# The first four expert tiles of a recurrence-and-router kernel loaded in rows and transposed by TensorE

## What is computed

```python
sig = 1.0 / (1.0 + np.exp(-f_logit))
f = lower_bound + (1.0 - lower_bound) * sig
for t in range(S):
    h = f[:, t] * h + (1.0 - f[:, t]) * x[:, t]
    y[:, t] = h
# router on y, as 20224 rows of 256
logits = normalized(y) @ normalized(expert_emb).T / tau
e = argmax(logits)
gate = softmax(logits)[e]
out = gate * (relu(y @ w1[e]) @ w2[e])    # w1: 256x1024, w2: 1024x256
```

## Time and profile before

| | us |
|---|---|
| median of three executions | 477.56 |
| lowest, highest of the three | 477.22, 479.57 |
| the profiled execution's own time | 479.34 |
| its span, first to last instruction | 477.5 |
| TensorE busy (93% of the span) | 442.5 |
| VectorE busy (75%) | 358.7 |
| GpSimd busy (70%) | 332.0 |
| ScalarE busy (68%) | 323.9 |

### The profile page before, as it was taken

How to read it: one execution, slowest core, us unless ns; L and a number is a source line. 1 busy time by engine, 2 the same in 40 slices (tenths; PEclk the granted TensorE clock), 3 DMA queues, 4 the chain that set the end, 5 groups by cost and what they waited for, 6 DMA issues and landing times. The chain is left out here.

```text
span 477.5 us, 12371 instructions
## 1 busy us (share of the span) xinstructions
PE 442.5 (93%) x4082; PEld 378.3 (79%) x4082; DVE 358.7 (75%) x1075; ACT 323.9 (68%) x567; POOL 332.0 (70%) x388
## 2 busy tenths in 40 slices
PE   7975868869999999999999999999999999999994
PEld 4554555657898888898887869999999999988993
DVE  6997899967999999999999999654455455444542
ACT  4886878975889989999988964444454454434441
POOL 8154657735777777777777777777777777777654
PEclk9998899997999999999999999999999999999998
DMA  7999999999999999999999654565554546455511
GB/s 235 310 330 316 256 317 327 216 220 312 306 258 295 277 304 295 288 326 259 289 262 225 141 125 115 143 145 130 133 126 124 132 108 134 113 141 138 110 63 67
DMA packets 122081, 100.44 MB, mean 210 GB/s; under 512 B 100052, under 2 KB 101087, under 8 KB 122016
## 3 DMA queue, kind: packets, MB, share of 16 engines
q1 hardware_dynamic: 104064, 59.33, 49.3%
q0 software_dynamic: 16224, 40.26, 31.9%
q10 hardware_dynamic: 1728, 0.01, 0.2%
HBM read 58.37 MB, written 32.93 MB: 191 GB/s over the span
## 5 line engine op out<-in xcount | busy, mean ns | idle before, releaser
L1465 POOL DMA_INDIRECT out_dram<-osb,xm x162 | 160.6, 992 | 63.3 <-issue 36.8
L1106 POOL DMA_INDIRECT XsScratch<-Yt,sli x158 | 152.3, 964 | 65.4 <-issue 23.8
L1440 PE MATMUL bank<-wall,hT 128*128 x1296 | 166.3, 273 | 1.1 <-DVE hb L837 0.8
L1392 PE MATMUL bank<-ys,wall 128*128 128x256 bf16 (+1 forms) x1392 | 164.7, 267 | 0.6 <-DVE osb L1459 0.3
L1392 PEld LDWEIGHTS bank<-ys,wall 128*128 x1392 | 147.3, 145 | 6.7 <-issue 1.7
L1440 PEld LDWEIGHTS bank<-wall,hT 128*128 128x128 bf16 x1296 | 125.1, 98 | 19.2 <-ACT fg L796 2.6
L1413 ACT ACTIVATE hT<-bank 128x512 bf16<-128x512 f32 x162 | 95.8, 597 | 59.3 <-PE bank L1392 52.0
L1418 DVE TENSOR_SCALAR hT<-bank 128x512 bf16<-128x512 f32 x162 | 110.5, 686 | 33.2 <-PE bank L1392 28.8
L837 DVE TENSOR_TENSOR_SCAN hb<-fg,hb,bank 128x512 f32<-128x512 f32 (+4 forms) x78 | 96.0, 1238 | 0.0
L1459 DVE TENSOR_SCALAR osb<-bank,xm 128x256 f32<-128x256 f32 x81 | 38.9, 480 | 58.7 <-ACT osb L1455 57.8
L1455 ACT ACTIVATE osb<-bank,xm 128x256 f32<-128x256 f32 x81 | 38.3, 473 | 44.3 <-PE bank L1440 32.8
(11 more groups left out here) (136 smaller groups left out, 296.6 us busy)
## 6 DMA issues: line engine op xcount, KB each, us to landing
fin<-in_f_logit_dram SPq DMA_DIRECT2D x39, 512.0 KB
xin<-in_x_dram SPq DMA_DIRECT2D x39, 512.0 KB
wall<-in_moe_w_dram POOLq DMA_DIRECT2D x16, 512.0 KB, 10.4
out_dram<-osb,xm POOLq DMA_INDIRECT x162, 2.8
XsScratch<-Yt,sli POOLq DMA_INDIRECT x158, 6.2
ys<-XsScratch SPq DMA_TRANSPOSE x87, 2.8
xm<-XsScratch SPq DMA_DIRECT2D x75, 2.0 KB
XsScratch<-nulr SPq DMA_DIRECT2D x8, 68.0 KB
```

Of the source, the lines that this page charges most:

```text
L1106: lambda e, j=o + j, i=o + k_ * 4 + b: e.indirect_dma_start(out=Xs[:, :], out_offset=bass.IndirectOffsetOnAxis(ap=sli[y][:, j : j + 1], axis=0
L1392: i = e.matmul(bank[hh[f // 2].b][:, at : at + R_], wall[:, bass.ds(a1[j, s][(4 * mp + f) * DT + kt] - WA - WREV, 2 * FT * P),].bitcast(BF ...
L1440: i = e.matmul(po(s), hT[qh][:, kf, s * P : (s + 1) * P], wall[:, bass.ds(a2[j, s if last else 0][kf] - WA, 2 * D)].bitcast(BF16), start=( ...
L1465: lambda e, s=s: e.indirect_dma_start(out=out[:, :], out_offset=bass.IndirectOffsetOnAxis(ap=xm[qx][:, s, 1:2], axis=0), in_=osb[qo][:, s, :],
```

## The change

For the first four tiles (`NPE = 4`) the DMA transpose into `ys` is left out. A plain load (`ldp`) reads the 256 rows whole, 544 bytes each, two neighbouring rows to a partition, into the tile's output buffer `osb`, which is free until the tile's end. TensorE then turns the bf16 features with four matmuls against the identity (`turn`: the data is the stationary operand, 128 x 128 each) into one bank of PSUM, and ScalarE copies the bank, 128 x 512, to `ys`. The load of gates and numbers (`ldm`) of these tiles lays row 2p + s at partition p, place s, to match. All tiles from 4 on are as before. As the recorded work differs, the scheduler orders all engines anew from there on.

```diff
+        NPE = 4
...
-                    Xs[bass.ds(evl[j, s], R_), P : P + 2].rearrange("(s p) r -> p s r", p=P),
+                    Xs[bass.ds(evl[j, s], R_), P : P + 2].rearrange(
+                        "(p s) r -> p s r" if j < NPE else "(s p) r -> p s r", p=P
+                    ),
+                )
+
+            def ldp(e):
+                r = reg(e, f"row{j}_0")
+                e.load(r, tbl[u][j : j + 1, 0:1])
+                r = evl[j, 0] = e.snap(r, donate=True, min_val=0, max_val=NULLROW)
+                return e.dma_start(
+                    osb[qo][:].rearrange("p s d -> p (s d)").bitcast(I32)[:, 0:RW],
+                    Xs[bass.ds(r, T), :].rearrange("(p s) r -> p (s r)", s=2),
                 )
...
                 lo = op(
+                    "sp", ldp, 950, r=rd, w=[("osb", qo, k) for k in range(2)],
+                    dma=f"xs{qy}", nbytes=140000,
+                ) if j < NPE else op(
...
+            if j < NPE:
+                hy = Hold("a")
+
+                def turn(e):
+                    for s in range(2):
+                        for kt in range(DT):
+                            at = kt * T + s * P
+                            i = e.matmul(
+                                bank[hy.b][:, at : at + P],
+                                osb[qo][:].rearrange("p s d -> p (s d)").bitcast(BF16)[
+                                    :, s * RW + kt * P : s * RW + (kt + 1) * P
+                                ],
+                                identb[:], start=True, stop=True,
+                            )
+                    return i
+
+                pe(
+                    turn, 300, r=[("osb", qo, 0), ("osb", qo, 1), "identb"], h=hy,
+                    deps=pr.readers.get(("ys", qy, 0), []), prio=EVP(pr.prio),
+                )
+                act(
+                    lambda e: e.activation(ys[qy][:], bank[hy.b][:], AF.Copy), 512, h=hy,
+                    w=[("ys", qy, 0), ("ys", qy, 1)], prio=EVP(pr.prio),
+                )
```

## The result

| | before | change |
|---|---|---|
| median, us (13 executions each) | 477.56 | 474.56 |
| lowest, highest | 474.78, 479.57 | 472.83, 476.52 |
| the profiled execution, its span | 479.34, 477.5 | 476.37, 474.6 |
| TensorE busy in the span | 442.5 | 438.5 |

The ratio of the change to the kernel before is 0.9947 (95% interval 0.9927 to 0.9968): faster by 1.5 to 3.5 us. The forecast was 473.7 us in 470.8 to 478.6, most likely faster.

What follows compares the result with a forecast made beforehand. TensorE was taken as full from 113 us, so time could be won only at the stall before it. 7.1 - 1.0 - 1.3 = 4.8 us off 479.34 gives 474.5, less half the 1.78 us excess: 473.7 us, range 470.8 to 478.6.

Steps and rivals of the forecast that it cites:

- The stall: After 102 us: TensorE's 4.55 us idle on chunk 16's `xin` and 2.54 us of slow clock go, together 7.1 us.
- The marks named for it: 95 to 125 us: no `xin` wait over 1 us; clock 1.00 from 95 us; no two-digit DMA rate while chunk loads wait.
- Halving the excess over the median: Profiled execution is 1.78 us above the median; half of that taken off, between 474.5 and 472.8, giving 473.7 us.
- The turns: First four tiles: 16 added matmuls on a full TensorE cost 1.0 us, at most 1.7; starts 60 to 110 ns apart.
- The copies: First four tiles: four ScalarE evictions at 597 ns cost 1.3 us, bounds 0 and 2.4; TensorE waits of 1 to 2 us.
- small terms: First four tiles: added costs set against the 7.1 us, 1.0 us for the turns and 1.3 us for the copies.
- GpSimd: No scatter added; it can start earlier and near the end waits for VectorE, so TensorE sets the end; no cost.
- The new order of the mixed part: After the start: the same work with TensorE full, costed at nothing.
- First output scatter some 5 us earlier: Sign of being right: GpSimd's first output scatter, at 108.92 us before after 6.14 us idle, starts some 5 us earlier.
- The jam that moves to tile 4: Rival: tiles 4 and 5's transposed loads hold up chunk 18's `xin`; half of 7.1 us lost, 477.3 us; chance 0.18.
- Transposed loads not the cause: Rival: weights and scatters jam, chunk 16's load stays late, the change only adds; 480.8 us; chance 0.09.
- ScalarE as the wait at the first four tiles: Rival: TensorE idles some 2.2 us per tile behind ScalarE's copies, 8.8 us instead of 1.3; 481.2 us; chance 0.07.

Runs made afterwards that it cites:

- plain_plus_T: The change plus an unused transposed load of the same rows behind each of the four plain loads: 482.08 us, 1.0103 of the kernel before.
- order_only: Kernel before, all loads transposed, first four planned at the plain loads' cost to give SyncE the change's order: 484.49 us, ratio 1.0117 to before.
- b_again: The kernel before, unchanged, one more profiled execution: 476.58 us.
- before_nx12: The kernel before with twelve instead of eight buffers for gates and token numbers, on a slower chip: 571.76 us, 0.9993 of the kernel before.
- npe2: The change with two tiles turned by TensorE instead of four: 479.02 us, 1.0008 of the kernel before.

## Why the prediction was right, and where it wasn't

- **The stall** (7.1 us off, all of it). The mechanism was right, and is shown from both sides: with transposed loads back in place the jam returns (`plain_plus_T`), with the order alone it doesn't go (`order_only`). The marks named for it came: no wait on `xin` from 95 to 125 us, the clock at 1.00 from 94 to 113, no window there under 229 GB/s. From trace to trace the early gain is that of the sum: 6.3 to 7.3 us of lead around 120 us, 4.3 to 5.3 without the 2.0 of the earlier start, against 4.8. The term may be too large for a usual execution: it was taken from a profiled execution of 479.34 us, and `b_again` loses 4.74 us in the same place, without the slow clock. Halving the excess over the median covered part of that.
- **The turns** (1.0 us). Measured 0.92 us; the starts are 58 ns apart, just under the 60 to 110 named. The Trainium skill (TensorE: Matmul & The Clock Gate, "Part 4: PE-mode transpose") gives about 275 ns for a transpose in one kernel; by it, as an estimate, the turns would take 4.4 us. The trace doesn't agree for turns that follow each other: one matmul of a turn takes 219 ns from start to end, near the page's figure, but the next one starts after 58. The page speaks of TensorE's transpose mode, and the turn is an ordinary matmul.
- **The copies** (1.3 us in the sum, 1 to 2 us of waits on ScalarE). TensorE's waits on ScalarE around the first tiles that are new come to some 0.3 us. The lower bound, "0 if TensorE has other work in its order", was the nearer one. In its place stands a wait that was not in the list: 1.2 us of the second turn on its plain load. The sum of the small terms came out near, 0.92 + 0.3 + 1.2 = 2.4 us instead of 2.3.
- **GpSimd** ("so that TensorE, not GpSimd, sets the end", and everything after 113 us at no cost). This step failed in part, and one sign of being wrong came with it: TensorE is no longer full between 113 and 440 us. GpSimd did get ahead and, by its n-th scatter of either kind, kept a lead of over 8 us from 120 to 430 us, 1.2 of them from before the first tile, yet TensorE's tile work kept only 5.7, and 2.5 us of that went where ScalarE stood behind GpSimd's scatter. I had asked whether GpSimd sets the end, and not who waits for its scatters on the way. The same load stood for 3.3 us in the trace of before too, from 419.58 on, where TensorE had enough in hand. The new order of the mixed part, costed at nothing, brought 1.8 us of short waits of TensorE by 160 us.
- **First output scatter some 5 us earlier.** It came 3.5 us earlier, and part of that is the earlier start of that execution (2.0 us on TensorE).
- **The rivals.** The jam that moves to tile 4: SyncE's issue of 4.27 us is there, the late chunk load isn't. The single later wait on a chunk load is 0.6 us. Transposed loads not the cause: refuted by `plain_plus_T`; but the weights, which that rival blamed, may be the other half of the cause, and I had not thought of both being needed. The Trainium skill (Advanced Engine Details and Errata, "X-Bar Transpose (TRN2)") has transposing DMAs as fast as regular ones; the 45 GB/s of `plain_plus_T` do not agree, and no run here compares the two kinds alone. ScalarE as the wait at the first four tiles: not there.

So the forecast was within 0.9 us with a gain that was 4.8 us in the sum and 3.0 in the medians: a stall taken from one execution, where another lost less, and a loss at 418 us that nobody had looked for. That it came so near is in part luck. With the 4.74 us of `b_again`, the 2.4 us of small terms and the 2.5 us lost at 418 us, nothing of the gain would be left, and yet the medians differ by 3.0: how a usual execution gains them isn't shown.

## What to carry to other kernels

When a load is late, read how long its queue's issues take and what the DMA moves at that moment: a high share with 45 to 95 GB/s named the jam here, and then changing the kind of load helped where changing its place in the queue made it worse. Take the size of a stall from two executions before it goes into a sum. And where work starts earlier, look at which buffers it asks for earlier: ScalarE, which issues its own loads near the end, stood 5.6 us at one that had to wait, and computed nothing meanwhile.

## What was not expected of the hardware

- Where the first tiles' transposed loads run beside the chunk and weight loads, the DMA's rate falls to 45 to 95 GB/s for about 4 us, at a share of 0.72 to 1.04 (`plain_plus_T` 45, before 49, `before_nx12` 62, `b_again` 83, `order_only` 95), and issuing a transposed load takes up to 7.78 us instead of 1.2. In the change, on either kind of chip, and in `npe2` no 4 us from 84 to 116 us are that low.
- The same program takes 478 us on one chip and 564 to 572 us on three others, with first-layer matmuls of 267 and 272 ns; a gain on the one need not be there on the others.
